# Handing the expert output to the MLP in on-chip memory, in expert order, in a fused attention, MoE and MLP kernel

## The chip, the cores and the metric

One Trainium2 chip, one core. The metric is the device time of one execution in microseconds (us), as the median of the timed runs. Engines: PE is TensorE (matmuls and transposes), ACT is ScalarE, DVE is VectorE, POOL is GpSimd, SP is SyncE. PEld is the weight load of TensorE, and a "q" behind an engine's name (ACTq) is its instruction sequencer, which works ahead of the engine.

## What is computed

```python
# x: (1152, 512), made by attention with queries averaged in pairs; batch b, position s is row 576*b + s
logits = x @ w_gate                       # 8 experts
e = argmax(logits); gate = softmax(logits)[e]
eom = sigmoid(x @ w_output_gate)[e]
y[e rows] = gate * eom * (relu(x[e rows] @ w1[e]) @ w2[e])      # w1: 512x1024, w2: 1024x512
h = y @ w_in                              # (1152, 2048)
out = (h * tanh(softplus(h))) @ w_out     # (1152, 512)
```

The dense MLP works on each row of `y` by itself, so the order of the rows is free as long as each result is written to its own row of `out`.

## The kernel before

**Attention** (up to about 290 us). Eight heads run in pairs, nine query tiles of 128 rows a head. The result, `x_tok`, is in token order. Meanwhile SP fills the DRAM buffer `slots_dram` with zeros and loads the weights of experts 0 and 1.

**Routing** (290 to 308.6 us). Logits, the chosen expert and each token's rank within its expert are worked out on PE and DVE. Every row is scaled by its gate and scattered by POOL (L677, one indirect DMA for each of the nine tiles) to its slot in `slots_dram`, where every expert begins on a tile boundary. DVE then works out how many tiles each expert has (`tile_end`, `bounds`) and at which row of `slots_dram` each tile lies (L1468 to L1476, `tile_rows`, semaphore `rows_ready`). After that it raises `h1_ready` (L1480), for which PE's first expert matmul waits. DVE's helper `then` lets each small operation wait for the one before it.

**Experts** (308.6 to 480.5 us). In this run 13 tiles of 128 slots are worked on, each with one expert's weights. `expert_tiles` (L451) is a loop of two groups of four experts, and inside it a loop over the tiles of each expert; four weight slots of 4 MB form the ring. Each step does:
- PE: first product into four PSUM banks, f = 0 to 7 (L995), then four transposes (`fill_xs`, L982) that turn the next tile, which lies in `stage`, into `turn[0]`, then the second product (L1009), f = 0 to 7, each f needing one eighth of w2 split into a high and a low part.
- ACT: ReLU to `hT_hi` (L1195) and the high part `w2_hi` (L1190) for f = 0 to 3 as they come, then `copy_xs` (L1179), then `w2_hi` for f = 4 to 7, then the DMA that loads `stage` for the tile after next (L1203).
- DVE: `hT_lo` (L1491), `w2_lo` (L1486), four of them late, and at the end the copy of the result to `y_sb` (L1500).
- POOL: writes `y_sb` back over the tile's own rows in `slots_dram` (L685) and waits for the landing.

SP loads each next expert when its ring slot is free (`wait_expert`, L578), then `w_in` (after expert 4) and `w_out` (after expert 5), 4 MB each.

**Hand-over** (480.5 to 518.5 us). When all tiles are stored, POOL gathers the rows back in token order, nine indirect DMAs (L691) into `x_tok`. ACT and DVE split `w_in` into high and low parts, four pieces of 2048 columns each (L1213, L1506). PE turns each gathered tile (`fill_x2`, L1020, four transposes), ACT and DVE split it into `x2T_hi` and `x2T_lo` (L1217, L1512). Three tiles come before the first MLP product, six between the first ones.

**MLP** (to the end). Three chunks of 384 rows, 16 steps each. A step f is `hidden` (L1032, 12 matmuls, run four steps ahead, `AHEAD`) and `project` (L1049, 9 matmuls). Between them lies the activation: ACT exp (L1222), ln (L1226), exp (L1228) and `g_hi` (L1234); DVE clip (L1520), L1522, L1539, L1542, L1534, L1548 and `g_lo` (L1527), which comes two DVE steps after its `hidden`. In chunk 0 each step also splits one sixteenth of `w_out` (L1256, L1576). PE's `hidden` waits for `h2_bank_free`, first raised by DVE at L1581. After a chunk, ACT (tiles 0 and 2) and DVE (tile 1) copy the result to `y_out`, and SP stores it (L603, L606; 128 KB twice for the last tile).

The lines on which the order hangs:

```python
            for n in range(RING):                      @@ SP
                wait_expert(n)
                load_expert(RING + n, n)
            wait_expert(RING)
            sp.dma_start(w_in_sb[:, :, :], w_in.rearrange("(t p) f -> p t f", p=P)).then_inc(w_in_landed, 16)
...
            pool.sem_inc(y_all_stored, 1)               # POOL
            pool.wait_ge(y_all_stored, 1)
            for i in range(TPH):
                pool.indirect_dma_start(x_tok[:, i, :], None, slots_dram,
                                        bass.IndirectOffsetOnAxis(slot_idx[:, i:i + 1], 0)).then_inc(y_back[i], 16)
```

Of the kernel before, what the change touches and what calls it, by code (L numbers as in the profile page):

```python
# [20 lines left out]
def build(nc, q, k, v, w_gate, w_ogate, w1, w2, w_in, w_out, out):  # L21
# [25 lines left out]
    XS_RING = 4  # L47
# [4 lines left out]
    DRAM_TILES = PAIRS * REGION // P  # L52
# [9 lines left out]
    FILL_STEPS = 3  # L62
# [9 lines left out]
    with ExitStack() as ctx:  # L72
# [18 lines left out]
        x_tok = sb("x_tok", [P, TPH, D], F32)  # L91
# [14 lines left out]
        row_step = sb("row_step", [P, NE], F32)  # L106
        row_base = sb("row_base", [P, NE], F32)
# [3 lines left out]
        tile_rows = sb("tile_rows", [P, ROW_TILES], I32)  # L111
        bounds = sb("bounds", [1, NE + 1], I32)
# [10 lines left out]
        parts_at = xsT_at + DT * N * 4  # L123
        ring = [ring_slot(n, at) for n, at in enumerate(ring_at)]

        w_in_sb = sb("w_in_sb", [P, DT, F2], F32, ring_at[0])
        w_in_lo = sb("w_in_lo", [P, DT, F2], F32R, ring_at[0])
        w_in_hi = sb("w_in_hi", [P, DT, F2], F32R, ring_at[2])
        w_out_sb = sb("w_out_sb", [P, FT2, D], F32, ring_at[1])
        w_out_lo = sb("w_out_lo", [P, FT2, D], F32R, ring_at[1])  # L130
        w_out_hi = sb("w_out_hi", [P, FT2, D], F32R, ring_at[3])
# [3 lines left out]
        xrT = sb("xrT", [P, DT, N], F32, ring_at[2])  # L135
        assert DT * N * 4 <= 2 * (B * KT * DH + TPH * 2 * DH) * 4
        x2T_hi = sb("x2T_hi", [P, DT, N], F32R, xsT_at)
        x2T_lo = sb("x2T_lo", [P, DT, N], F32R, xsT_at + DT * N * 4)
        stage = sb("stage", [P, FILL_AHEAD + 1, D], F32, xsT_at + DT * XS_RING * P * 4)

# [7 lines left out]
        y_out = sb("y_out", [P, TC, D], F32, x_tok_at)  # L148
        g_at = x_tok_at + TC * D * 4
        g_hi = sb("g_hi", [P, 2, CW], F32R, g_at)  # L150
        g_lo = sb("g_lo", [P, 2, CW], F32R, g_at + 2 * CW * 4)
        mish_at = [xsT_at + 2 * DT * N * 4]
# [15 lines left out]
        assert mish_at[0] <= top_at and g_at + 4 * CW * 4 <= x_tok_at + 2 * TC * D * 4  # L168

        small_from = xsT_at + DT * XS_RING * P * 4 + (FILL_AHEAD + 1) * D * 4  # L170
# [29 lines left out]
        row_of = small("row_of", [ROW_TILES, NE])  # L200
# [3 lines left out]
        raw_k = sb("raw_k", [P, 2, KT, B, DH], F32)  # L204
        raw_q = sb("raw_q", [P, 2, TPH, 2 * DH], F32)
# [8 lines left out]
        q_turned = sb("q_turned", [P, Q0 * P], F32)  # L214
        q_hi = sb("q_hi", [P, Q0 * P], F32R)
        q_lo = sb("q_lo", [P, Q0 * P], F32R)
        kT = sb("kT", [P, 2, B * S], F32R)
        qT_at = cursor[0]
        qT = sb("qT", [P, 2, 2, TPH * P], F32R)
        scratch = [sb(f"scratch{n}", [P, P], F32, x_tok_at + n * P * 4) for n in range(2)]  # L220
        prob = sb("prob", [P, 2, S], F32)
        probT = sb("probT", [P, 4, S], F32)
# [10 lines left out]
        assert qT_at <= small_from and small_at[0] <= qT_at + 2 * 2 * TPH * P * 4  # L233

        fill_bank = turn
        x2_fill_bank = [turn[0], turn[1], pvT]
# [40 lines left out]
        stage_landed = [sem(f"stage_landed{n}") for n in range(FILL_AHEAD + 1)]  # L277
# [7 lines left out]
        y_sb_free = sem("y_sb_free")  # L285
        s2_done = sem("s2_done")
        y1_copied = sem("y1_copied")
        y_stored = sem("y_stored")
        y_all_stored = sem("y_all_stored")
        y_back = [sem(f"y_back{n}") for n in range(TPH)]  # L290
        w_in_landed = sem("w_in_landed")
        w_out_landed = sem("w_out_landed")
# [8 lines left out]
        h2_bank_free = sem("h2_bank_free")  # L301
        g_ready = sem("g_ready")
        y2_done = sem("y2_done")
        y2_copied_act = sem("y2_copied_act")
# [390 lines left out]
        def _(pe):  # L695
# [364 lines left out]
            for i in range(TC):  # L1060
                fill_x2(i)
# [549 lines left out]
```

## Time and profile before

| | us |
|---|---|
| median of 3 runs | 721.02 (720.47 to 721.58) |
| profiled execution, its own time | 717.5 |
| its span (first to last instruction) | 715.9 |
| PE busy | 676.5 (94%) |
| DVE busy | 505.1 (71%) |
| ACT busy | 405.6 (57%) |
| POOL busy | 90.8 (13%) |
| mean granted clock of TensorE | 0.981 |

All positions in the trace are us from the start of the span. The profiled execution is 3.5 us shorter than the median of the runs. A duration printed for a matmul is longer than the distance to the next one, as matmuls overlap; the distance between starts is what they cost. Overlapping operations of DVE and ACT, too, follow each other some 0.07 to 0.09 us closer than their durations say.

### The profile page before, as it was taken

The numbers are of one execution on the slowest core, as the hardware profiler recorded it, in microseconds if no ns is written. First come the engines' busy times: TensorE is split into PE (matmuls) and PEld (weight loads), VectorE is DVE, ScalarE is ACT, GpSimd is POOL, SyncE is SP. The second block draws the span as 40 slices with busy tenths as digits, with TensorE's granted clock in tenths as the row PEclk, the third lists the DMA queues.
The fourth block names the chain that finished last, engine by engine and source line by source line (L and its number), as shares of the span: only waits on it lengthen the run. The fifth ranks groups of instructions, "written<-read, shape, count | busy, mean of one in ns | idle before, by whom it ended". The sixth has DMA issues, their size and how long they took to land.

```text
span 715.9 us, 14780 instructions
## 1 busy us (share of the span) xinstructions
PE 676.5 (94%) x5169; PEld 597.5 (83%) x5170; DVE 505.1 (71%) x1157; ACT 405.6 (57%) x810; POOL 90.8 (13%) x123
## 2 busy tenths in 40 slices
PE   5999999999999999989999999983799999999997
PEld 5788888888888888789998999973689998999895
DVE  5767676777677776756566566556899978777875
ACT  4657565756666667346555556653666645455442
POOL 2303040404041200320000000006000000000000
PEclk9899999999999999999999999995999999999999
DMA  7578989796977500389963991014000010001001
GB/s 190 142 204 221 279 206 262 172 260 153 256 165 203 133 3 1 99 310 402 399 246 121 349 347 47 29 48 128 15 1 1 1 44 1 1 0 45 1 1 44
DMA packets 92385, 99.00 MB, mean 138 GB/s; under 512 B 41584, under 2 KB 65136, under 8 KB 91824
## 3 DMA queue, kind: packets, MB, share of 16 engines
q1 hardware_dynamic: 87536, 86.22, 40.9%
q0 software_dynamic: 2480, 8.13, 3.2%
q10 hardware_dynamic: 2320, 4.00, 1.7%
q8 instruction: 30, 0.49, 0.3%
q14 instruction: 19, 0.16, 0.1%
HBM read 62.16 MB, written 19.66 MB: 114 GB/s over the span
## 4 chain that ended last, share of the span: by engine, by line
PE 89%; DVE 5%; ACT 2%; DMA 2%; issue 1%; POOL 1%; SPq 0%; ACTq 0%; POOLq 0%; DVEq 0%
PE score_banks L1032 14%; PE score_banks L995 13%; PE turn L782 12%; PE pvT L763 11%; PE score_banks L1009 10%; PE score_banks L739 5%; PE score_banks L740 5%; PE score_banks L1049 4%; PE turn L1049 4%; PE pvT L1049 4%; PE turn L703 1%; PE turn L982 1%; DMA raw_k<-k 1%; POOL x_tok L691 1%; PE turn L789 1%
## 5 line engine op out<-in xcount | busy, mean ns | idle before, releaser
L782 PE MATMUL turn<-ident,prob 128*128 128x128 f32 x648 | 111.5, 282 | 2.4 <-DVE x_tok L1330 0.5
L1277 DVE TENSOR_REDUCE nmax_part<-score_banks 128x1 f32<-128x768 f32 x72 | 68.9, 957 | 60.3 <-PE score_banks L740 46.9
L995 PEld LDWEIGHTS score_banks<-xsT,w_slot 128*128 128x128 f32 x832 | 94.6, 192 | 5.2 <-issue 4.2
L995 PE MATMUL score_banks<-xsT,w_slot 128*128 x832 | 95.2, 275 | 3.6 <-DVEq L1480 2.0
L782 PEld LDWEIGHTS turn<-ident,prob 128*128 128x128 f32 x648 | 77.5, 142 | 24.9 <-issue 14.0
L1078 ACT ACTIVATE prob<-score_banks,nmax 128x1152 f32<-128x1152 f32 x72 | 87.5, 1215 | 0.6 <-DVE nmax L1287 0.5
L1085 ACT ACTIVATE probT<-turn 128x384 f32<-128x384 f32 x72 | 35.4, 491 | 89.3 <-PE turn L782 89.3
L763 PE MATMUL pvT<-probT,v_sb 128*64 128x128 f32 (+1 forms) x1404 | 85.9, 269 | 0.0
L1486 DVE TENSOR_TENSOR w_lo<-w_slot,w_hi 128x512 fp32r<-128x512 f32 x104 | 71.7, 692 | 18.5 <-ACT w_hi L1190 18.4
L739 PE MATMUL score_banks<-kT,qT 128*128 128x384 f32 x192 | 80.1, 417 | 4.6 <-DVE qT L1306 3.9
L763 PEld LDWEIGHTS pvT<-probT,v_sb 128*64 128x64 f32 x1404 | 69.5, 137 | 11.8 <-issue 11.8
L1032 PE MATMUL score_banks<-x2T_hi,w_in_hi 128*128 128x384 f32 x192 | 66.1, 344 | 4.3 <-DVE x2T_lo L1512 4.3
L1195 ACT ACTIVATE hT_hi<-score_banks 128x128 fp32r<-128x128 f32 x104 | 28.8, 277 | 69.4 <-PE score_banks L995 64.6
L1190 ACT ACTIVATE w_hi<-w_slot 128x512 fp32r<-128x512 f32 x104 | 65.3, 628 | 2.1
L740 PE MATMUL score_banks<-kT,qT 128*128 128x384 f32 x192 | 65.7, 342 | 0.0
L1032 PE MATMUL score_banks<-x2T_hi,w_in_lo 128*128 128x384 f32 x192 | 65.5, 341 | 0.0
L1032 PE MATMUL score_banks<-x2T_lo,w_in_hi 128*128 128x384 f32 x192 | 65.2, 340 | 0.0
L1234 ACT ACTIVATE g_hi<-prod 128x384 fp32r<-128x384 f32 x48 | 25.3, 526 | 62.2 <-PE turn L1049 55.4
L1491 DVE SCALAR_TENSOR_TENSOR hT_lo<-score_banks,hT_hi 128x128 fp32r<-128x128 f32 x104 | 29.9, 287 | 30.0 <-ACT hT_hi L1195 30.0
L1527 DVE TENSOR_TENSOR g_lo<-prod,g_hi 128x384 fp32r<-128x384 f32 x48 | 26.7, 557 | 23.9 <-ACT g_hi L1234 22.3
L739 PEld LDWEIGHTS score_banks<-kT,qT 128*128 128x128 f32 x192 | 36.8, 192 | 7.1 <-DVE qT L1306 4.4
L1032 PEld LDWEIGHTS score_banks<-x2T_hi,w_in_hi 128*128 128x128 f32 x192 | 36.6, 191 | 7.0 <-DVE x2T_lo L1512 5.0
(218 smaller groups left out, 1358.0 us busy)
## 6 DMA issues: line engine op xcount, KB each, us to landing
w_slot<-moe_w SPq DMA_DIRECT2D x16, 2048.0 KB, 15.7
slots_dram<-zeros SPq DMA_DIRECT2D x8, 1408.0 KB, 11.1
raw_k<-k SPq DMA_DIRECT2D x16, 288.0 KB, 5.9
v_sb<-v SPq DMA_DIRECT2D x16, 288.0 KB, 4.3
w_in_sb<-moe_w_in SPq DMA_DIRECT2D x1, 4096.0 KB, 13.7
w_out_sb<-moe_w_out SPq DMA_DIRECT2D x1, 4096.0 KB, 14.6
kT<-k_hi SPq DMA_DIRECT2D x14, 288.0 KB, 4.3
kT<-k_lo SPq DMA_DIRECT2D x14, 288.0 KB, 5.2
```

The source lines that it names most:

```text
L739: pe.matmul(dst, parts(0, P), keys(b), start=True, stop=False)
L740: last = pe.matmul(dst, parts(1, P), keys(b), start=False, stop=True)
L763: last = pe.matmul(bank[half * DH:(half + 1) * DH, col:col + cols], v_sb[:, par, j, b, :], probT[:, pt_of[t], j * P + col:j * P + col + cols],
L782: last = pe.transpose(bank[:, j * P:(j + 1) * P], prob[:, s % 2, c * KC + j * P:c * KC + (j + 1) * P], ident[:, :])
L995: last = pe.matmul(h1_bank[f % 4][:, 0:P], w1_e[:, d, f * P:(f + 1) * P], xsT[:, d, bass.ds((t % XS_RING) * P, P)], start=(d == 0), stop=( ...
L1009: last = pe.matmul(y1_bank, h, w, start=(f == 0 and k == 0), stop=(f == FT1 - 1 and k == 2))
L1032: last = pe.matmul(h2_bank[f % 4][:, 0:CW], w, x, start=(d == 0 and k == 0), stop=(d == DT - 1 and k == 2))
L1049: last = pe.matmul(y2_bank[n], g, w, start=(f == 0 and k == 0), stop=(f == FT2 - 1 and k == 2))
L1078: act.activation(prob[:, s % 2, :].rearrange("p (c n) -> p c n", c=NC), scores[s % 2][:, :, 0:KC], ACT.Exp, bias=nmax[:, s:s + 1], accum_o ...
L1190: act.activation(w2_hi[:, f % W2_RING, :], ring[n][1][:, f, :], ACT.Copy).then_inc(w2_hi_ready, 1)
L1277: dve.tensor_reduce(nmax_part[:, s, 0:1], scores[s % 2][:, lo:lo + 2, 0:KC], AX.XY, ALU.max, negate=True).then_inc(max_part, 1)
L1486: dve.tensor_tensor(w2_lo[:, f % W2_RING, :], ring[n][1][:, f, :], w2_hi[:, f % W2_RING, :].bitcast(F32), ALU.subtract).then_inc(w2_lo_rea ...
```

## The change

After each expert tile the result `y_sb` is no longer written to DRAM. One tile later PE turns it (`turn_y`, four transposes into `turn[1]`), ACT and DVE split it into `x2T_hi` and `x2T_lo` at the column at which the tile's first row stands when all rows are sorted by expert (`tile_cols`); padding rows behind it are overwritten by the next tile. The MLP then runs on rows in expert order, and its results are scattered to the rows of `out` by POOL. The row numbers are worked out in chunk 1 of the MLP: DVE makes 0/1 matrices (`spread`), PE multiplies them with the row numbers (`gather_rows`, nine matmuls with nine columns), DVE copies them to `out_idx`. The experts are written out one by one. `w_in` and `w_out` are loaded in halves into the freed halves of four ring slots, and six of eight pieces of `w_in` (two 512-column stretches at a time) are split behind experts 5, 6 and 7, the last two in steps 0 and 1 of chunk 0. Raising `h2_bank_free` now stands on DVE behind the pieces that follow expert 7 and a register load of the number of tiles. In the routing, four operations of 128x144 elements and one reduction of these leave; seven of at most nine elements, four of 72, two of 288, one of 36, two small stores and the clearing of `y_sb` come, all ahead of `h1_ready`. At the start POOL makes six more small tables. In the last chunk ACT and DVE copy tiles 0 and 1 as soon as each is done (`y2_tile_done`). The loop over the MLP's middle chunk, which runs once, is written out.

```diff
-    XS_RING = 4
+    XS_RING = 2
...
+        first_pieces = {RING + 1: ((0, 0), (0, 1)), RING + 2: ((1, 0), (1, 1)), RING + 3: ((0, 2), (1, 2))}
+        late_pieces = ((0, 3), (1, 3))
+        PIECES_READY = (3, 4, 6, 8)
...
-            with eng.Fori(0, NE // RING) as grp:
...
+            for e in range(NE):
+                with eng.Fori(firsts[e], firsts[e + 1]) as t:
+                    body(t, e, look_ahead)
+                if behind is not None:
+                    behind(e)
@@ SP
-            sp.dma_start(w_in_sb[:, :, :], w_in.rearrange("(t p) f -> p t f", p=P)).then_inc(w_in_landed, 16)
...
+            for n in range(2):
+                wait_expert(RING + n)
+                sp.dma_start(w_in_sb[n][:, :, :], w_in_rows[:, n * HALF:(n + 1) * HALF, :]).then_inc(w_in_landed[n], 16)
+            for n in range(2):
+                wait_expert(RING + 2 + n)
+                sp.dma_start(w_out_sb[n][:, :, :], w_out_rows[:, n * HALF2:(n + 1) * HALF2, :]).then_inc(w_out_landed[n], 16)
@@ POOL
-            with pool.Fori(0, tiles) as t:
-                pool.dma_start(slots_dram[bass.ds(row, P), :], y_sb[:, :]).then_inc(y_stored, 16)
...
+            pool.wait_ge(order_ready, 1)
+            for i in range(TPH):
...
+                pool.indirect_dma_start(out, bass.IndirectOffsetOnAxis(out_idx[:, i:i + 1], 0),
+                                        y_out[:, i % TC, :], None).then_inc(out_landed, 16)
@@ PE
+            def turn_y(t):
+                pe.wait_ge(y1_copied, t + 1)
+                pe.wait_ge(x2_lo_ready, t + 1)
+                for d in range(DT):
+                    last = pe.transpose(x2_bank[:, d * P:(d + 1) * P], y_sb[:, d * P:(d + 1) * P], ident[:, :])
+                last.then_inc(x2_filled, 1)
...
                 pe.wait_ge(xs_copied, t + FILL_AHEAD)
...
-                pe.wait_ge(y1_copied, t + 1)
+                turn_y(t)
...
-            for i in range(TC):
-                fill_x2(i)
-            pe.wait_ge(x2_lo_ready, TC)
-            pe.wait_ge(win_lo_ready, DT)
-            for f in range(AHEAD):
-                hidden(0, f)
-                for i in later_fills[f]:
-                    fill_x2(i)
-            pe.wait_ge(x2_lo_ready, TPH)
+            pe.wait_ge(x2_lo_ready, tiles + 1)
+            hidden(0, 0)
+            turn_y(tiles)
+            for f in range(1, AHEAD):
+                hidden(0, f)
...
+                    if c == 1:
+                        for i in spread_in(f + 1):
+                            gather_rows(i)
@@ ACT
                 copy_xs(t + FILL_AHEAD, fill_bank[0], (t + FILL_AHEAD) % XS_RING)
+                x2_high(t)
                 for f in range(W2_RING, FT1):
                     w2_high(f)
...
+            def x2_high(t):
+                col = act.value_load(tile_cols[0:1, bass.ds(t, 1)], min_val=0, max_val=N)
+                act.wait_ge(x2_filled, t + 1)
+                act.activation(x2T_hi[:, :, bass.ds(col, P)], x2_bank[:, :].rearrange("p (d n) -> p d n", d=DT), ACT.Copy
+                               ).then_inc(x2_hi_ready, 1)
@@ DVE
+            dve.memset(y_sb[:, :], 0.0).then_inc(y1_copied, 1)
+            dve.sem_inc(x2_lo_ready, 1)
             dve.sem_inc(h1_ready, 4)
...
                 look_ahead(e)
+                x2_low(t)
                 for f in range(W2_RING, FT1):
                     w2_low(f)
                 dve.wait_ge(s2_done, FT1 * (t + 2))
-                dve.wait_ge(y_sb_free, t + 1)
+                dve.wait_ge(x2_filled, t + 1)
                 dve.tensor_copy(y_sb[:, :], y1_bank).then_inc(y1_copied, 1)
@@ PE, project
+                    if c == CHUNKS - 1 and f == FT2 - 1 and n < TC - 1:
+                        last.then_inc(y2_tile_done, 1)
```

## Rows read from the trace of the kernel before

**Rows 1.** Busy time by engine, granted clock and DMA in the stretch of the hand-over.

```profile
480.50:518.50 38.00, 19.00 (x98) 16.93 (x98) 26.29 (x37) 20.18 (x30) 13.05 (x10) 0.78 0.24 71
```

**Rows 2.** Timeline of PE, hand-over: start us, us, line, operation, [idle before <-releaser].

```profile
480.14 0.39 PE L1009 MATMUL score_banks<-w_hi,hT_lo 128*128 128x512 f32 x1
490.85 1.11 PE L1020 MATMUL turn<-ident,x_tok 128*128 128x128 f32 x4 [10.32 <-DMA x_tok<-slots_dram,slot_idx]
...
497.70 0.69 PE L1032 MATMUL score_banks<-x2T_hi,w_in_hi 128*128 128x384 f32 x1 [1.41 <-DVE x2T_lo L1512]
...
516.30 0.45 PE L1032 MATMUL score_banks<-x2T_hi,w_in_hi 128*128 128x384 f32 x1 [2.91 <-DVE x2T_lo L1512]
...
518.50 0.39 PE L1049 MATMUL score_banks<-w_out_hi,g_hi 128*128 128x512 f32 x1
```

**Rows 3.** Windows of 1 us in the hand-over; PEclk is the granted clock.

```profile
484.00:485.00 1.00, 0.00 (x0) 0.00 (x0) 1.00 (x1) 1.00 (x2) 0.00 (x0) 0.73 0.00 0
501.00:502.00 1.00, 1.00 (x7) 0.96 (x7) 0.00 (x0) 0.11 (x1) 0.00 (x0) 0.73 0.78 209
```

**Rows 4.** The chain that ended last: start us, us, what.

```profile
387.26 1.58 issue
...
485.40 3.11 POOL x_tok L691
```

**Rows 5.** Timeline inside one expert tile.

```profile
381.17 0.60 PE L982 MATMUL turn<-ident,stage 128*128 128x128 f32 x4
...
381.53 0.48 PE L1009 MATMUL score_banks<-w_hi,hT_hi 128*128 128x512 f32 x1
...
383.18 2.08 DVE L1486 TENSOR_TENSOR w_lo<-w_slot,w_hi 128x512 fp32r<-128x512 f32 x3 [1.20 <-ACT w_hi L1190]
...
384.38 0.39 PE L1009 MATMUL score_banks<-w_hi,hT_hi 128*128 128x512 f32 x1
```

**Rows 6.** Groups of instructions: out<-in, shapes xcount | busy us, mean ns | idle before.

```profile
L1506 DVE TENSOR_TENSOR w_in_lo<-w_in_sb,w_in_hi 128x2048 fp32r<-128x2048 f32 x4 | 8.9, 2286 | 1.8 <-ACT w_in_hi L1213 1.8
...
L1213 ACT ACTIVATE w_in_hi<-w_in_sb 128x2048 fp32r<-128x2048 f32 x4 | 7.3, 1897 | 2.7 <-DMA stage<-slots_dram 2.7
...
L1512 DVE TENSOR_TENSOR x2T_lo<-turn,x2T_hi 128x512 fp32r<-128x512 f32 x6 | 4.0, 686 | 3.3 <-ACT x2T_hi L1217 3.3
...
L1217 ACT ACTIVATE x2T_hi<-turn 128x512 fp32r<-128x512 f32 x6 | 3.4, 588 | 5.2 <-PE turn L1020 5.2
```

**Rows 7.** The line that loads a tile's row number into a register, on ACT's sequencer.

```profile
L1202 ACTq TENSOR_LOAD <-tile_rows x13: 278/279/288, 319.3 to 477.9; - x13
```

**Rows 8.** Timeline of DVE, first steps of the MLP.

```profile
502.42 0.36 DVE L1520 TENSOR_SCALAR expo<-expo 128x384 f32<-128x384 f32 x1 [4.77 <-ACT expo L1222]
...
511.76 0.35 DVE L1520 TENSOR_SCALAR expo<-expo 128x384 f32<-128x384 f32 x1
...
512.63 0.55 DVE L1527 TENSOR_TENSOR g_lo<-prod,g_hi 128x384 fp32r<-128x384 f32 x1
```

**Rows 9.** Groups on DVE in the routing.

```profile
L1474 DVE TENSOR_TENSOR row_of<-row_of,begun 128x144 f32<-128x144 f32 x1 | 0.3, 309 | 0.0
...
L1416 DVE SCALAR_TENSOR_TENSOR gain_inv<-picked,gate_sum 128x4 f32<-128x4 f32 (+1 forms) x2 | 0.3, 160 | 0.0
```

**Rows 10.** Timeline of PE at the start of the experts.

```profile
299.19 7.39 PE L937 MATMUL score_banks<-onehot,x_tok 128*128 128x128 f32 x64
308.60 0.59 PE L995 MATMUL score_banks<-xsT,w_slot 128*128 x3 [2.02 <-DVEq L1480]
```

**Rows 11.** Timeline at the end of the kernel.

```profile
711.08 0.60 ACT L1241 ACTIVATE y_out<-score_banks 128x512 f32<-128x512 f32 x1 [3.04 <-PE turn L1049]
...
712.55 1.18 SPq L606 DMA_DIRECT2D out<-y_out  x2
```

**Rows 12.** Issue to landing of the last tile's stores from SP, L606.

```profile
DMA to landing us min/median/max: 2.4/2.4/2.4
```

**Rows 13.** Issue to landing of the indirect DMAs from POOL, L691.

```profile
DMA to landing us min/median/max: 3.5/3.8/5.4
```

More of the change, by code:

```diff
@@ L276, in build @@
         xs_stored = sem("xs_stored")
-        stage_landed = [sem(f"stage_landed{n}") for n in range(FILL_AHEAD + 1)]
+        stage_landed = sem("stage_landed")
         xs_filled = sem("xs_filled")
@@ L1012, in _ @@
             expert_tiles(pe, pe_expert)
-            def fill_x2(i):
-                pe.wait_ge(y_back[i], 16)
-                if i >= 3:
-                    pe.wait_ge(x2_lo_ready, i - 2)
-                bank = x2_fill_bank[i % 3]
-                for d in range(DT):
-                    last = pe.transpose(bank[:, d * P:(d + 1) * P], x_tok[:, i, d * P:(d + 1) * P], ident[:, :])
-                last.then_inc(x2_filled, 1)
+            tiles = pe.value_load(bounds[0:1, NE:NE + 1], min_val=NE, max_val=SLOT_TILES)
             def hidden(c, f):
                 pe.wait_ge(h2_bank_free, FT2 * c + f + 1)
+                if isinstance(c, int) and c == 0 and f % RANGE == 0:
+                    pe.wait_ge(win_lo_ready, PIECES_READY[f // RANGE])
                 cols = bass.ds(c * CW, CW)
                 for d in range(DT):
-                    wh, wl = (w[:, d, f * P:(f + 1) * P] for w in (w_in_hi, w_in_lo))
+                    wh, wl = (w[d // HALF][:, d % HALF, f * P:(f + 1) * P] for w in (w_in_hi, w_in_lo))
                     xh, xl = x2T_hi[:, d, cols], x2T_lo[:, d, cols]
@@ L1247, in mlp_chunk @@
                     rough_recip(c, f)
-                    if first:
-                        for i in later_fills[f]:
-                            x2_high(i)
                     if f + 1 < FT2:
@@ L1260, in mlp_chunk @@
                         g_high(c - 1, FT2 - 1, False)
-            for i in range(TC):
-                x2_high(i)
-            act.wait_ge(w_out_landed, 16)
             h2_exponential(0, 0)
+            x2_high(tiles)
             for c in range(CHUNKS):
@@ L1393, in sign_slots @@
                 tiles, count = slice(batches[n].start, batches[n].stop), len(batches[n])
-                then(dve.tensor_tensor(signed[:, tiles, :], chosen[:, tiles, :], spread(slot_sign[:, :], count, NE), ALU.mult))
+                then(dve.tensor_tensor(signed[:, tiles, :], chosen[:, tiles, :], spread_over(slot_sign[:, :], count, NE), ALU.mult))
             def pick(n):
@@ L1551, in copy_y @@
             def copy_y(c):
-                dve.wait_ge(y2_done, FT2 * (c + 1))
+                if c == CHUNKS - 1:
+                    dve.wait_ge(y2_tile_done, 2)
+                else:
+                    dve.wait_ge(y2_done, FT2 * (c + 1))
                 dve.wait_ge(y_out_free, c + 1)
@@ L1559, in mlp_chunk @@
                     mish_numer(c, f)
+                    if first and not f:
+                        x2_low(tiles)
                     if f >= 2:
```

355 lines of the change are left out of this document (215 added, 140 removed).

## The prediction, made before the changed kernel was run

> **What bounds the kernel now.** I read the busy shares first: PE is at 94%, so time is to be found where PE waits. The busy time by stretch shows one place: in the 38.0 us of the hand-over PE is busy for 19.0, at a mean clock of 0.78 [rows 1]. The timeline of PE tells what it waits for [rows 2]. The last expert matmul starts at 480.14, the first transpose of a gathered tile at 490.85, after 10.32 us that ended with a DMA; the first MLP matmul starts at 497.70, the first `project` at 518.50. Stand-alone windows show the clock: 0.73 from 484 to 485, so it fell from 2.4 to 1.2 GHz some 0.5 us into that window, 3.9 us after the last matmul ended at 480.53; again 0.73 from 501 to 502, so it rose near 501.5, after 3.8 us of dense matmuls [rows 3]. Elsewhere PE works back to back, in the experts and in the MLP, and everything added to PE there counts in full. The chain of waits adds two things [rows 4]: POOL's first gather (3.11 us), and 1.58 us of "issue" at 387.26, after the sixth expert tile, where the loop over groups of experts jumps back.
>
> **What the change removes, up to the first `project`.** I build its new start from the front.
>
> *Start of the experts.* PE ended at 299.19 + 7.39 = 306.58 and waited until 308.60 for DVE's `h1_ready` [rows 10]. That increment now stands behind more routing work. By the groups on DVE [rows 9] an operation of a few elements takes 0.16 and one of 144 takes 0.31, each about 0.04 more with its wait; so 0.20, about 0.26 for 72 elements, 0.50 for 288, 0.24 for 36. Added: 7 x 0.20 + 4 x 0.26 + 2 x 0.50 + 0.24 + 0.2 for two small stores = 3.9. Removed: 5 x 0.35 = 1.7. Sum **+2.2** (1.7 to 2.9; the upper end if the clearing of `y_sb` must end, too, at L1512's length [rows 6]). The six POOL tables cost nothing: the first use of the tables is hundreds of us later, and POOL's next work at the start waits for a DMA; without that cover, six small operations are 1.2.
>
> *Transposes.* `fill_xs` takes 381.53 - 381.17 = 0.36 for its four [rows 5]; `turn_y` has the same four, in 13 tiles: **+4.7**. Its input was copied a whole first product before, so PE doesn't wait for it. Behind it, ACT's x2 split (0.59) and DVE's (0.69) [rows 6] now stand ahead of the late parts of w2. The cover: the first late `w2_lo` starts at 383.18 and takes 0.69, done at 383.87; PE needs it at 384.38 [rows 5]. That is 0.51 minus some semaphore time, say 0.45. `turn_y` gives PE's need 0.36 more. ACT's part delays the split by 0.59; DVE's then ends just behind ACT's next w2 part. About 0.2 us of cover is left, so I cost it at nothing. The column load into a register (0.28 [rows 7]) can run while `copy_xs` runs; if not, it uses that cover up.
>
> *Loop written out.* The jump back between the groups goes: **-1.6** (0 if something else, such as loading code, takes its place).
>
> *Pieces of w_in.* A split of 2048 columns takes 1.90 on ACT and 2.29 on DVE [rows 6]; between the 512 and the 2048 rows, 1024 takes 1.05 and 1.22. After experts 5 and 6 DVE does two of them (2.4) at the head of the next tile. PE's fifth bank use waits for the first `hT_lo` only four products later, 3.6 us; that nearly covers it: **+0.2** (0 to 0.8). The loads of 2 MB have a whole tile to land.
>
> So the last expert matmul's slot, 480.37 before, ends at 480.37 + 2.2 + 4.7 - 1.6 + 0.2 = 485.9.
>
> *First MLP product.* PE now needs only `h2_bank_free`. ACT's two pieces end about 0.7 after the last product; DVE's sequencer then queues the last split, loads the number of tiles (0.28 plus handling) and raises it. I take 1.6 (0.6 if only the load counts; 3.5 if `y_sb`'s copy and both splits had to end first). First `hidden` at 487.5.
>
> *From there to `project`.* A `hidden` at full clock takes 518.50 - 516.30 = 2.2 [rows 2]. Then come 0.1 and ACT's exp, about 0.6 by the nearest row, to DVE's clip: 2.9. From the first clip to the end of the first `g_lo` it was 512.63 + 0.55 - 502.42 = 10.8 [rows 8]. In these two steps four x2 splits (4 x 0.69) go, one (0.69) and two pieces of w_in (2 x 1.22) come, +0.4, and each piece waits for ACT's 1.05 where a 0.59 stood, +0.8. So 2.9 + 10.8 + 1.2 + 0.1 = 15.0 and `project` starts at 502.5, not 518.50: **-16.0**. Here PE has only five `hidden` and one `turn_y` to do, 11 us, and waits 4.0; the DVE chain is the late one now.
>
> **What it adds behind.** *Row numbers:* nine small matmuls with a full weight load each; L937 has 64 such pairs in 7.39, 0.115 each [rows 10], so **+1.0** (0.4 to 1.7). DVE's part is hidden, since DVE is 71% busy and two steps ahead. *Last store:* SP issued the second part of the last tile at about 713.14, and it landed 2.4 later [rows 11, 12], 4.5 us after the copies began at 711.08. Now the third indirect DMA starts at about 712.95 (POOL, 1.25 apart, from the first copy, which comes some 0.7 earlier, three matmuls of 0.24 [rows 5]), and lands 3.5 later [rows 13]: **+0.9** (-0.4 if POOL is free at the last copy, +2.8 at the longest landing). A page speaks against moving this: the Trainium skill, "DMA: Bandwidth & Descriptors", section "Specifications", gives about 1 us to the first byte for a DMA issued by GpSimd and 0.6 from the sync path. By its difference alone the last landing would be 0.4 later, where the rows here make it 1.1.
>
> **Clock.** PE now waits 4.2 us before the first expert product (306.58 to 310.8) and 4.0 before the first `project`. The only fall in a wait here came after 3.9. A fall costs half of 3.8 us = 1.9. Both waits lie at the edge; I count one fall: **+1.9** (0 to 3.8).
>
> **Sum.** -16.0 + 1.0 + 0.9 + 1.9 = -12.2 against the profiled execution's 717.5 us: 705.3. The median shown is 3.5 us above that execution; against it, 721.0 - 12.2 = **708.8 us**.
>
> **The rivals.**
> - *Half clock at both edges, or a longer chain.* The trace speaks for it with the half clock from 484.5 to 501.5; against it, waits of 2.02 and 2.91 us [rows 2, 10] before matmuls at full speed. Two falls: 710.7. With the first product released only at 3.5, another 1.9: 712.6. The Trainium skill, "TensorE: Matmul & The Clock Gate", section "HAM oscillation — how this bites in real kernels", has every repeated wait for data throttle the array again and charges half of the throttled time; by that rule this is the likely outcome, and the one fall seen here agrees with it.
> - *No fall, and the DVE chain shorter than laid out.* 706.9 without a fall; down to 703 if the pieces of w_in overlap the activation better than I have it.
> - *Code loading.* If the 1.58 us stays although the loop is gone, 710.4. If each new expert's code costs it, 7 x 1.58 more, 721. Against it: experts 1 to 3 were entered for the first time without a wait in the chain.
> - *Slower.* In every tile the two x2 splits stand between `copy_xs` and the late w2 parts. If the register loads aren't hidden (0.28 and as much handling on each queue), and both splits lie in the chain in full, that is 0.59 + 0.69 + 1.2 = 2.5 against a cover of 0.45 + 0.36 = 0.8: 1.7 a tile, 13 tiles, +22, so 731. It decides from 12.2/13 = 0.94 us a tile. Against it: the two queues run beside each other, and DVE is idle for 1.20 ahead of the first late `w2_lo` [rows 5].
> - *It doesn't do what it says.* If the MLP's start were held by the splits of w_in or the activation chain as long as before, the gather's wait would have been cover only, and the 7 us added would show: 722 or so. Against it: 10.32 us of the wait end with the DMA [rows 2].
>
> **How the numbers follow.** Forecast, one fall give or take half of one: 0.48. Both falls or a longer chain, 710.5 to 714: 0.22. Better, 703 to 707: 0.19. Code loading of a part: 0.04. Slower: 0.04. No real effect: 0.03. The first three give the range, 703.0 to 714.0, which also takes in the bounds of start (+0.7), release (+1.9) and landing (+1.9) one at a time. A measurement of this kernel can tell about 0.2% (1.4 us) from no change. Faster by more than that 0.93, within 0.02, slower 0.05.
>
> **What would show it.** In the changed profile: the first L995 matmul near 310.8; each tile 0.36 longer than before, with no wait of PE between `turn_y` and the second product; no "issue" after the sixth tile; the first MLP product 1.6 us after the last expert one; then about 4 us of waiting for `g_lo` and `project` at 503 to 505; nine small matmuls in chunk 1 without waits; about 5.4 us from the last matmul's release to the end. Wrong would be: tiles over 0.94 longer, a wait of over 4 us before the first MLP product, or more than two stretches at half clock.

## The result, and the profile after

The changed kernel takes **710.27 us** (median of 4 runs, 709.43 to 712.92) beside 721.3 us for the kernel before: 11.0 us less, a ratio of 0.9848 [0.9814, 0.9882]. The forecast was 708.8 with a range of 703.0 to 714.0, so sign and time were right. Its case, one fall of the clock, was not: there are two. The time came out by luck: terms that were too small by 6.5 us in all were made up for by the executions that the sum was measured against. The rest of this text takes that apart.

| | before | changed |
|---|---|---|
| profiled execution, own time | 717.5 | 712.92 |
| its span | 715.9 | 711.2 |
| mean granted clock | 0.981 | 0.988 |
| last expert matmul starts | 480.1 | 492.9 |
| first `hidden` | 497.7 | 494.4 |
| first `project` | 518.5 | 509.4 |

The head of the page, changed kernel (share of the span):

```profile
PE 681.7 (96%) x5207; PEld 601.9 (85%) x5207; DVE 509.8 (72%) x1193; ACT 408.2 (57%) x819; POOL 80.9 (11%) x115
```

PE has 5 us more work than before and the kernel is shorter all the same. The timeline of PE, changed kernel, at the start of the experts and in the hand-over (start us, us, instruction, [idle before <-releaser]), answers to [rows 2, 10]:

```profile
312.82 0.79 PE L1035 MATMUL score_banks<-xsT,w_slot 128*128 x2 [3.95 <-ACT xsT L1218]
...
494.41 0.41 PE L1066 MATMUL score_banks<-x2T_hi,w_in_hi 128*128 128x384 f32 x1 [1.16 <-DVEq L1596]
...
509.45 0.76 PE L1083 MATMUL score_banks<-w_out_hi,g_hi 128*128 128x512 f32 x1 [3.93 <-DVE g_lo L1607]
510.01 0.63 PE L1083 MATMUL score_banks<-w_out_lo,g_hi 128*128 128x512 f32 x1
```

The wait of 10.32 us for the gathered rows is gone; what is left before the first MLP product is 1.16 us, until DVE's register load, and the DVE chain to `g_lo` is the late one from there on, as laid out: 15.04 us from the first `hidden` to the first `project`. The windows of the changed kernel (the column behind POOL's is the granted clock) show what the two long waits bring:

```profile
310.00:311.00 1.00, 0.00 (x0) 0.00 (x0) 0.93 (x3) 0.00 (x0) 0.99 (x1) 1.00 1.02 414
311.00:312.00 1.00, 0.00 (x0) 0.00 (x0) 0.86 (x8) 0.09 (x1) 0.13 (x1) 0.60 1.04 422
312.00:313.00 1.00, 0.18 (x1) 0.19 (x2) 0.76 (x3) 0.51 (x1) 0.00 (x0) 0.50 0.86 348
...
317.00:318.00 1.00, 1.00 (x7) 1.00 (x6) 0.77 (x2) 0.43 (x1) 0.00 (x0) 0.50 0.85 252
318.00:319.00 1.00, 1.00 (x11) 1.00 (x11) 0.44 (x2) 0.73 (x2) 0.00 (x0) 0.99 0.87 242
...
509.00:510.00 1.00, 0.55 (x1) 0.50 (x2) 1.00 (x3) 0.97 (x3) 0.00 (x0) 0.59 0.00 0
510.00:511.00 1.00, 1.00 (x4) 0.80 (x3) 1.00 (x3) 0.93 (x3) 0.00 (x0) 0.50 0.00 0
...
512.00:513.00 1.00, 1.00 (x4) 0.76 (x4) 0.96 (x3) 0.33 (x1) 0.00 (x0) 0.71 0.00 0
513.00:514.00 1.00, 1.00 (x7) 0.96 (x7) 1.00 (x4) 0.97 (x3) 0.00 (x0) 1.00 0.00 0
```

Both waits of about 4 us let the clock fall from 2.4 to 1.2 GHz: at the start of the experts it stays down until 318 (11 matmuls a us instead of 7 from there), at the first `project` until about 512.6. The 17 us at half clock of [rows 3] are gone.

One tile, changed kernel (timeline), answers to [rows 5]:

```profile
390.86 0.60 PE L1013 MATMUL turn<-ident,stage 128*128 128x128 f32 x4
391.30 0.60 PE L1022 MATMUL turn<-ident,y_sb 128*128 128x128 f32 x4
391.65 0.47 PE L1049 MATMUL score_banks<-w_hi,hT_hi 128*128 128x512 f32 x1
...
392.37 0.60 ACT L1232 ACTIVATE x2T_hi<-turn 128x512 f32 x1
392.86 2.45 ACT L1241 ACTIVATE w_hi<-w_slot 128x512 fp32r<-128x512 f32 x4
...
393.12 0.69 DVE L1556 TENSOR_TENSOR x2T_lo<-turn,x2T_hi 128x512 f32 x1 [1.45 <-ACT x2T_hi L1232]
393.72 2.48 DVE L1564 TENSOR_TENSOR w_lo<-w_slot,w_hi 128x512 fp32r<-128x512 f32 x4
...
394.26 0.39 PE L1049 MATMUL score_banks<-w_hi,hT_lo 128*128 128x512 f32 x1
394.55 0.47 PE L1049 MATMUL score_banks<-w_hi,hT_hi 128*128 128x512 f32 x1
394.86 0.39 PE L1049 MATMUL score_banks<-w_lo,hT_hi 128*128 128x512 f32 x1
```

`fill_xs` to `turn_y` is 0.44 here, not 0.36, `turn_y` to the second product 0.35. The 13th matmul of the second product comes 0.29 behind the 12th and the 14th 0.31 behind that, where nearly all others are 0.23 apart: the first late `w2_lo`, 393.72 to 394.4, is just too late. So the cover of the x2 splits had not 0.2 us left but was 0.06 short, and being 0.06 short costs 0.14. The chain of the changed kernel around that tile:

```profile
383.88 7.14 PE score_banks L1035 x64
391.03 0.44 PE turn L1013 x4
391.46 0.44 PE turn L1022 x4
391.90 5.65 PE score_banks L1049 x24
397.55 7.14 PE score_banks L1035 x64
```

Tile follows tile after 13.67 us (13.07 before), with no piece of "issue" between them, behind the sixth either. That 1.58 us [rows 4] is gone.

The routing on DVE, changed kernel, with ACT's first copy:

```profile
307.42 0.16 DVE L1521 CAST bounds<-tile_end 1x9 int32<-1x9 f32 x1
...
309.84 0.46 DVE L1535 TENSOR_TENSOR begins_at<-begun,starts_of 128x288 f32<-128x288 f32 x1
310.33 0.45 DVE L1537 TENSOR_REDUCE tile_at_f<-begins_at 128x36 f32<-128x288 f32 x1
...
312.15 0.16 DVE L1547 TENSOR_TENSOR out_row_f<-out_row_f,tail_part 128x1 f32<-128x1 f32 x1
312.48 0.48 DVE L1549 MEMSET y_sb<- 128x512 f32 x1 [0.17 <-DVE out_row_f L1547]
...
311.91 0.60 ACT L1218 ACTIVATE xsT<-score_banks 128x512 f32<-128x512 f32 x1 [11.32 <-remote]
```

One of the row products in chunk 1, and the end of the kernel (timeline of the changed kernel):

```profile
583.99 0.39 PE L1083 MATMUL turn<-w_out_hi,g_lo 128*128 128x512 f32 x1
584.22 0.28 PE L1091 MATMUL turn<-rows_by_tile,spread 128*128 128x9 f32 x2
584.36 0.42 PE L1066 MATMUL score_banks<-x2T_hi,w_in_hi 128*128 128x384 f32 x1
584.61 0.34 PE L1066 MATMUL score_banks<-x2T_lo,w_in_hi 128*128 128x384 f32 x1
...
703.13 0.60 ACT L1298 ACTIVATE y_out<-score_banks 128x512 f32<-128x512 f32 x1 [1.71 <-PE score_banks L1083]
...
704.00 0.96 POOL L721 DMA_INDIRECT out<-y_out,out_idx  x1 [54.81 <-ACT y_out L1298]
...
705.27 0.96 POOL L721 DMA_INDIRECT out<-y_out,out_idx  x1 [0.30 <-issue]
706.53 0.96 POOL L721 DMA_INDIRECT out<-y_out,out_idx  x1 [0.30 <-issue]
```

Each fp32 product of nine columns is two passes (x2), and delays the work behind it by 584.61 - 584.22 - 0.18 = 0.21 us. At the end POOL is the bound, 1.26 us a DMA, and the third one needs another 4.7 us to the end of the span at 711.2.

### The profile page after: what moved, and what is told of

It is laid out like the page before. It is cut to its first block, busy times and chain, and to the rows that moved or that the text cites. A ratio compares the mean times of both kernels' runs of the same rounds, so it can differ in the third digit from the quotient of the medians.

```text
span 711.2 us, 14872 instructions
## 1 busy us (share of the span) xinstructions
PE 681.7 (96%) x5207; PEld 601.9 (85%) x5207; DVE 509.8 (72%) x1193; ACT 408.2 (57%) x819; POOL 80.9 (11%) x115
## 4 chain that ended last, share of the span: by engine, by line
PE 89%; DVE 4%; ACT 2%; another core or an unknown queue 2%; issue 1%; DMA 1%; POOL 0%; DVEq 0%; SPq 0%; ACTq 0%
PE score_banks L1035 13%; PE score_banks L1066 13%; PE turn L813 11%; PE pvT L794 11%; PE score_banks L1049 10%; PE score_banks L770 5%; PE score_banks L1083 5%; PE score_banks L771 5%; PE pvT L1083 4%; PE turn L1083 4%; PE turn L734 1%; DMA raw_k<-k 1%; PE turn L1022 1%; PE turn L1013 1%
## 5 line engine op out<-in xcount | busy, mean ns | idle before, releaser
L1035 PEld LDWEIGHTS score_banks<-xsT,w_slot 128*128 128x128 f32 x832 | 97.1, 196 | 5.2 <-issue 4.1
L1035 PE MATMUL score_banks<-xsT,w_slot 128*128 x832 | 97.5, 279 | 3.9 <-ACT xsT L1218 3.9
L794 PEld LDWEIGHTS pvT<-probT,v_sb 128*64 128x64 f32 x1404 | 69.5, 137 | 11.9 <-issue 11.9
L1564 DVE TENSOR_TENSOR w_lo<-w_slot,w_hi 128x512 fp32r<-128x512 f32 x104 | 68.2, 687 | 3.0 <-ACT w_hi L1241 2.9
L1241 ACT ACTIVATE w_hi<-w_slot 128x512 fp32r<-128x512 f32 x104 | 63.5, 625 | 0.7
L721 POOL DMA_INDIRECT out<-y_out,out_idx x9 | 8.9, 991 | 387.4 <-DVE out_idx L1688 308.9
L1049 PE MATMUL score_banks<-w_hi,hT_hi 128*128 128x512 f32 x104 | 42.8, 411 | 0.0
```

The lines of the kernel that those rows point to most:

```text
L794: last = pe.matmul(bank[half * DH:(half + 1) * DH, col:col + cols], v_sb[:, par, j, b, :], probT[:, pt_of[t], j * P + col:j * P + col + cols],
L1035: last = pe.matmul(h1_bank[f % 4][:, 0:P], w1_e[:, d, f * P:(f + 1) * P], xsT[:, d, bass.ds((t % XS_RING) * P, P)], start=(d == 0), stop=( ...
L1049: last = pe.matmul(y1_bank, h, w, start=(f == 0 and k == 0), stop=(f == FT1 - 1 and k == 2))
L1241: act.activation(w2_hi[:, f % W2_RING, :], ring[n][1][:, f, :], ACT.Copy).then_inc(w2_hi_ready, 1)
L1564: dve.tensor_tensor(w2_lo[:, f % W2_RING, :], ring[n][1][:, f, :], w2_hi[:, f % W2_RING, :].bitcast(F32), ALU.subtract).then_inc(w2_lo_rea ...
```

## The experiments

Each ratio is against the kernel before, run beside the experiment. The first four (the kernel without the gather, late pieces, splits behind, no row products) ran on one chip, the others in two sets on another. No changed kernel ran beside the first four; I compare them with its 710.27 of the result, whose chip is not on record (the kernel before took 721.3 us beside it and 721.05 beside the four), so differences of 1 to 2 us there are weak. The others have a repeat of the changed kernel beside them, 709.47 and 710.51.

**The gather alone.** The kernel before without its nine gathers; `x_tok` keeps what it held, so the MLP works on other rows of data, in the same shapes.

```diff
-            for i in range(TPH):
-                pool.indirect_dma_start(x_tok[:, i, :], None, slots_dram, ...)
...
-                pe.wait_ge(y_back[i], 16)
...
+            dve.wait_ge(y_all_stored, 1)
             dve.sem_inc(h2_bank_free, 4)
```

> The kernel before without the nine gathers and without PE's wait for them: the MLP gets the scaled inputs in token order instead of the experts' output; the stores of the expert output stay. Theory (the round trip is only a part; the splits of w_in and their place on ACT and DVE are the next bound): DVE ends the last w_in split where it did, about 11.5 us after the last expert matmul, then does three x2 splits, so the first MLP matmul comes about 13.6 us after the last expert matmul instead of 17.2, and the kernel is 3 to 4 us faster than before (717 to 718 against 721). Rival (the round trip is the whole of the 10.3 us wait and its clock): first MLP matmul within 5 us, 10 to 13 us faster.

Measured: 719.77 us (10 runs), ratio 0.9982 [0.9962, 1.0002]: 1.3 us less, by the interval between 2.7 less and no gain, although 10.32 us of waiting ended with those gathers. That is also less than the 3 to 4 us expected. Its timeline:

```profile
497.95 0.69 PE L1028 MATMUL score_banks<-x2T_hi,w_in_hi 128*128 128x384 f32 x1 [12.14 <-DVE x2T_lo L1508]
```

The wait moved to DVE, which had the splits of `w_in` ahead of the x2 splits. The first `hidden` comes 13.8 us after the last expert matmul instead of 17.6, as expected, but from it to `project` it is 22.4 instead of 20.8, with one more stretch at half clock behind a wait of 2.99 us: the hand-over is 2.1 us shorter in all. **The gather was a cover for the splits of w_in,** and taking it away alone brings next to nothing.

**The other half alone.** The changed kernel with all six early pieces of `w_in` behind expert 7.

```diff
-first_pieces = {RING + 1: ((0, 0), (0, 1)), RING + 2: ((1, 0), (1, 1)), RING + 3: ((0, 2), (1, 2))}
+first_pieces = {RING + 3: ((0, 0), (0, 1), (1, 0), (1, 1), (0, 2), (1, 2))}
```

> The changed kernel with all six early pieces of w_in split behind expert 7 instead of behind experts 5, 6 and 7. Theory: four more pieces on ACT (about 0.96 us each) stand ahead of the release of the first MLP matmul, so PE waits about 1.1 + 4 = 5 us there instead of 1.1, with a fall of the clock on top (1.7 to 2): 4 to 6 us slower than the changed kernel, which was 710.3. Rival (w_in's splits don't matter, the removal of the round trip alone made the gain): within 1 us of it.

Measured: 715.15 us (5 runs), ratio 0.9921 [0.9891, 0.9951], 4.9 over the changed kernel.

```profile
497.07 0.66 PE L1066 MATMUL score_banks<-x2T_hi,w_in_hi 128*128 128x384 f32 x1 [4.94 <-DVEq L1596]
```

The wait before the first `hidden` is 3.8 longer, and its products run at half clock: 16.85 instead of 15.04 us to `project`. So the gain of the change is made of both parts: rows that stay on chip, and pieces of `w_in` that are split under the experts.

**x2 splits behind the late w2 parts**, on ACT and DVE.

```diff
                 copy_xs(t + FILL_AHEAD, fill_bank[0], (t + FILL_AHEAD) % XS_RING)
-                x2_high(t)
                 for f in range(W2_RING, FT1):
                     w2_high(f)
+                x2_high(t)
```

> The changed kernel with the two x2 splits of each expert tile moved behind the late parts of w2 on ACT and DVE. Theory (the tile costs 0.61 us more than before, 0.36 of it the four transposes, and the rest because the late w2 parts come later than PE needs them): the gap of 0.31 between the 12th and 13th matmul of the second product falls back to 0.23, a tile takes 13.07 + 0.36 to 13.07 + 0.45, and the kernel is 2 to 3 us faster than the changed one. Rival (the extra 0.25 is PE's own cost of two transposed tiles in a row with their waits): 13.65 a tile, no change.

Measured: 710.25 us (4 runs), ratio 0.9853 [0.9835, 0.9871]. The tile is 13.49 instead of 13.66 and the gap in it is gone, so the x2 splits did cost 0.17 a tile where they stood. But the two tiles that begin with pieces of `w_in` on ACT and DVE take 13.75, and behind the last tile the splits now delay the last pieces:

```profile
490.67 0.41 PE L1066 MATMUL score_banks<-x2T_hi,w_in_hi 128*128 128x384 f32 x1 [2.08 <-DVEq L1596]
```

From the second tile to the last expert matmul 1.6 us come in (not 13 x 0.17 = 2.2), and 0.9 go out; the median shows no difference from the changed kernel's. In the pair with and without the move that the other chip ran (below) it is -2.0.

**No row products** (the results are then written in expert order, not to their own rows; the nine 0/1 matrices on DVE are left out, too).

```diff
-                        for i in spread_in(f + 1):
-                            gather_rows(i)
...
-                    dve.tensor_copy(out_idx[:, :], x2_bank[:, 0:TPH])
+                    dve.tensor_copy(out_idx[:, :], out_row_f[:, :])
```

> The changed kernel without the nine 0/1 matrices and the nine products; the results are scattered by the unsorted row numbers, so rows of the output land in other places, with the same stores. Theory: each product costs PE 0.19 us; the nine steps of chunk 1 take 4.19 instead of 4.39 us, 1.7 us less in all. Rival (the products fill gaps that stay): no change in the steps.

Measured: 708.72 us (4 runs), ratio 0.9839 [0.9815, 0.9863]. From the first `project` to the last matmul it is 192.7 us beside 194.6 with the products: 1.9 for nine, 0.21 each.

**The changed kernel again**, as yardstick.

> The changed kernel once more, beside the next three: 709.4 to 712.9 were measured. Its first expert tile took 16.4 us instead of 13.3 in the trace of before, and so did the kernels of the first call, the one built on the kernel before too (15.7): theory, the half clock at the start of the experts is common to both kernels in most runs. Then this trace shows it again (a first tile of 15.5 us or more). Rival: it was chance, and some traces show 13.7.

Measured: 709.47 us (5 runs), ratio 0.988 [0.9852, 0.9909]; kernel before 718.21 (11 runs).

```profile
311.58 2.71 PE L1035 MATMUL score_banks<-xsT,w_slot 128*128 x11 [3.78 <-DVEq L1551]
```

ACT's copy was done at 308.4 here, and the wait ends with the increment at the end of the routing, 5.3 us after `bounds` (3.5 before). The first tile takes 16.48 us, the later ones about 13.66: **the fall costs 2.8 us** in this profile.

**The release right behind the bounds.**

```diff
             dve.tensor_copy(bounds[0:1, :], tile_end[0:1, :]).then_inc(bounds_ready, 1)
+            dve.sem_inc(h1_ready, 4)
...
+            dve.sem_inc(rows_ready, 1)
             dve.memset(y_sb[:, :], 0.0).then_inc(y1_copied, 1)
...
-            dve.sem_inc(h1_ready, 4)
@@ ACT
-            act.wait_ge(rows_ready, 1)
+            act.wait_ge(rows_ready, 2)
```

> The changed kernel with the release of the first expert product right behind the tile counts, some 4.7 us earlier in DVE's work; ACT waits for the rest of the routing instead, before it writes over the small tables. Theory (DVE's longer routing is the bound of the start): PE starts the experts about 0.3 us after ACT's first xsT copy, 2 to 3 us earlier after the tile counts than the 5.3 us of the changed kernel, and if the wait falls under 3 us the clock doesn't fall (2.4 more): 2 to 5 us faster than the changed kernel. Rival (ACT's late copy of the first tile, which the trace puts down to an unknown queue, is as late as DVE): PE starts less than 0.5 us earlier, no change.

Measured: 706.24 us (6 runs), ratio 0.984 [0.9814, 0.9867], 3.2 less than the changed kernel beside it.

```profile
307.85 3.83 PE L1035 MATMUL score_banks<-xsT,w_slot 128*128 x32 [1.37 <-ACT xsT L1218]
...
311.68 0.28 ACT L1246 ACTIVATE hT_hi<-score_banks 128x128 fp32r<-128x128 f32 x1 [4.57 <-PE score_banks L1035]
...
312.33 4.07 PE L1035 MATMUL score_banks<-xsT,w_slot 128*128 x32 [0.66 <-DVE hT_lo L1570]
```

PE starts 2.9 us after `bounds`, behind ACT's copy, and the clock stays at 1.00. Yet the first tile takes 15.15 us, not 13.66. The edit also makes ACT wait for the end of the routing (`rows_ready`); ACT loads the tile counts only from 310.1 on and begins `hT_hi` at 311.68. PE has filled its four banks by then and waits for the `hT_lo` behind it. So 2.4 us come from the earlier start and 1.3 from the first tile, and 0.35 are lost in the third tile (14.00; why stays open): 3.4 in all, near the 3.2 of the medians. The longer routing still costs time in this version, through ACT.

**The same, with the load of the next w1 held back** until the first copy is done, to see if that load makes ACT's copy late.

```diff
+            sp.wait_ge(xs_copied, 1)
```

> The kernel with the early release, and with the 2 MB load of expert 2's first weights held back on SP until ACT has copied the first tile. Theory (ACT's first xsT copy is late by 2 to 3 us because what it waits for, its instructions by the look of it, comes by DMA behind that load and the scatters): ACT copies within 0.3 us of the last product of the placing, PE starts the experts about 1 us after it, at full clock: a first tile of 13.7 us, and 4 to 5 us faster than the changed kernel. Rival (the lateness has nothing to do with the load): ACT is as late as before, the same time as the kernel with the early release alone.

Measured: 711.03 us (6 runs), ratio 0.9905 [0.988, 0.9931]. ACT's copy came right behind the last product of the routing, but so it did beside it without this wait: no answer. The run is 4.8 us slower. In its profile, 2.6 of that lie between `bounds` and the second tile, as the load of `stage` now lands late and PE waits 2.35 us for it, and 1.3 at the first `project`, where the clock stays at half for 6.8 us instead of 3.4.

**A warm clock at the first project:** 18 matmuls more, whose result nobody reads, while PE waits for `g_lo`.

```diff
+                    if first and f == 0:
+                        pe.wait_ge(x2_lo_ready, tiles + 2)
+                        for _ in range(18):
+                            pe.matmul(x2_bank[:, 0:CW], w_in_hi[0][:, 0, 0:P], x2T_hi[:, 0, 0:CW], start=True, stop=True)
                     project(c, f, first)
```

> The changed kernel with 18 more matmuls of 384 columns (their result is not used) between PE's fifth hidden product and the first project, 3.1 us in the 3.9 us that PE waits there. Theory (the half clock at the first project comes from that wait): it stays at full clock, the first project takes 2.1 instead of 3.6 us, 1.5 us faster than the changed kernel. Rival (the clock falls for another reason, or the added matmuls push the project back): no gain, or up to 0.5 us slower.

Measured: 707.31 us (5 runs), ratio 0.9853 [0.9824, 0.9883], 2.2 less than the changed kernel beside it.

```profile
505.30 0.47 PE L1083 MATMUL score_banks<-w_out_hi,g_hi 128*128 128x512 f32 x1 [0.83 <-DVE g_lo L1611]
```

The first `project` takes 2.1 us instead of 3.6: 1.5, as expected, which shows that the fall there comes from the wait. The rest of the gain need not be the edit's. Counted from `bounds` to the end, this profile is 2.6 us shorter than that of the changed kernel, and 1.05 of it lies in the first expert tile (15.43 instead of 16.48, same order of work), where the clock happened to come back sooner.

**Put together.** The yardstick, then early release and warm clock, then these and the splits behind.

> The changed kernel once more, as the yardstick of this call. Expected 709.5 +- 1 by the median, first tile of the experts 16.4 to 16.7, tiles of 13.66 after it, first hidden matmul to first project matmul 15.0.

> The release right behind the bounds and the matmuls that keep the clock, together. If the two costs are separate, the gains add: 3.2 and 2.2 below the changed kernel of the same call, so about 704.1. If one only uncovers the other (a fall that is avoided at one place comes at the next), it stays at 706 to 707.

> As the run with the early release and the kept clock, and the splits of x2 behind those of w2 as well. By my reading the tiles shrink from 13.66 to 13.49 (13 x 0.17 = 2.2) and the first hidden matmul waits 1.1 longer: net 1.1 below the kernel without the move. The rival: the wait grows by as much as the tiles give, and the two are equal within 0.3.

Measured, with the kernel before at 717.25 beside them (9 runs):

| | us (runs) | ratio to before |
|---|---|---|
| changed again | 710.51 (5) | 0.9906 [0.9889, 0.9923] |
| early, warm | 706.40 (4) | 0.9859 [0.9839, 0.9878] |
| early, warm, splits behind | 704.38 (5) | 0.9821 [0.9804, 0.9839] |

Early release and warm clock bring 4.1 us by the medians, between the 3.2 of the first alone and the 5.4 of both added. The profiles tell more: from `bounds` to the end the pair is 4.9 us shorter than the changed kernel, which is 3.4 for the release and 1.5 for the warm `project`, so the two add up. The profile of this pair has no half clock from the start of the experts to the last matmul. The version with all three beats both kernels of this case: 6.1 us under the changed one, 2.0 under the pair. Its profiled execution had no luck at one place; its timeline and its windows there:

```profile
487.76 0.41 PE L1066 MATMUL score_banks<-x2T_hi,w_in_hi 128*128 128x384 f32 x1 [2.08 <-DVEq L1601]
```

```profile
487.00:488.00 1.00, 0.24 (x1) 0.27 (x2) 1.00 (x2) 0.01 (x1) 0.00 (x0) 1.00 0.75 186
488.00:489.00 1.00, 1.00 (x5) 1.00 (x5) 0.67 (x1) 0.00 (x0) 0.00 (x0) 0.57 0.79 150
489.00:490.00 1.00, 1.00 (x5) 1.00 (x4) 0.00 (x0) 0.00 (x0) 0.00 (x0) 0.50 0.96 326
```

The same wait of 2.08 us that let the clock be in the run with the splits behind alone was followed by a fall here, and `project` came 16.6 us after the first `hidden` instead of 15.0.

## Why the prediction was right, and where its terms were off

The sum was made against a profiled execution of 717.5 us, so it is checked against one of the changed kernel with the same start of the attention, that of the first repeat (span 710.2; 715.9 before). Each row is a distance between two events in the two traces:

| stretch | before | changed | found | predicted |
|---|---|---|---|---|
| start to `bounds` | 305.1 | 306.3 | +1.2 | 0 |
| `bounds` to first expert matmul | 3.5 | 5.3 | +1.8 | +2.2 |
| first tile | 13.2 | 16.5 | +3.3 | +0.4, and +1.9 once for a fall |
| the other tiles, to the last matmul | 158.4 | 163.8 | +5.4 | +2.9 |
| to the first `hidden` | 17.6 | 1.6 | -16.0 | -15.7 |
| to the first `project` | 20.8 | 15.0 | -5.8 | -5.8 |
| to the last matmul | 192.1 | 194.6 | +2.5 | +1.0 |
| to the end | 5.3 | 7.2 | +1.9 | +0.9 |
| sum | | | -5.7 | -12.2 |

- **What made the kernel faster was right to 0.3 us:** the hand-over (-21.8 for -21.5). The release after the register load came out as summed (1.56 for 1.6), and so did the chain of DVE in its parts: 2.96 to the first clip (2.9), 11.9 from there to the end of the first `g_lo` (12.0).
- **Start of the experts.** +1.8 for +2.2, within its bounds. That clearing `y_sb` must end was wrong: in the changed kernel PE's first matmul starts at 312.82, with the MEMSET under way until 312.96.
- **Transposes, the term that was mis-sized most.** 0.60 a tile instead of 0.36, so 13 x 0.60 = 7.8 for 4.7. 0.08 lies between `fill_xs` and `turn_y`, 0.14 to 0.17 at the second product's late matmul. The step that failed is "about 0.2 us of cover is left, so I cost it at nothing": moving the splits away gave back 0.17 a tile, so the cover was used up. It also shows that the rival "slower" had the right place; it needed 0.94 a tile and got 0.60.
- **Loop written out.** -1.6 was right: no "issue" is left between the tiles, and no other piece took its place; the rival of code loading is out. The +0.2 for the pieces of `w_in` was not needed: the tiles behind them take 13.66 and 13.68, like the others.
- **Clock.** "Both waits lie at the edge; I count one fall" is the step that failed. Both fell in every profile of the unaltered changed kernel: 2.6 to 2.8 us in the first tile and 1.5 at `project` (its first step takes 5.7 us instead of 4.2), 4.3 for the 1.9 of the forecast. The rival "half clock at both edges" (0.22) names what happened, with 710.7 against the 710.27 measured. The rule of the Trainium skill, "TensorE: Matmul & The Clock Gate", section "HAM oscillation — how this bites in real kernels", that every repeated wait throttles again, gave the outcome here where I rated it as the less likely; the runs bound it from the other side, since waits of 1.16, 1.37 and 2.35 us let the clock be.
- **Row products.** 1.9 for 1.0. The sum took a single pass of 0.115 each; each product is two, and the matmul behind them is late too. Without them the stretch is 1.9 us shorter.
- **Last store.** +1.9 for +0.9. The third DMA starts 2.5 after the last matmul (2.35 forecast; two slips cancel there: against the last matmul the first copy came 1.34 earlier than before, not 0.7, since six matmuls and not three lie behind its tile, and the 0.6 that the copy itself takes were left out). It needs about 4.3 to land (an estimate: 4.7 less the 0.4 that lay between landing and end before), not the 3.5 taken from [rows 13]. The difference to SP's 2.4 is 1.9. "DMA: Bandwidth & Descriptors" of the Trainium skill, section "Specifications", gives 1 us and 0.6 us to the first byte for the two paths, 0.4 apart. Here the stores differ in size and kind as well (256 KB indirect, 128 KB plain), so no run shows what share of the 1.9 is the path's.
- **Not foreseen.** MLP steps take 4.186 us instead of 4.207, 48 of them -1.0; why stays open. `bounds` came 1.2 to 2.3 us later than before in the three profiles of the unaltered changed kernel, but not in most of the edited ones (303.4 to 306.2), so I take it for scatter between executions.

By this table the sum was 6.5 us too hopeful, and yet 708.8 stands 1.5 from the measured median. The rest is the yardstick. The profiled execution of the kernel before was 3.5 us under its median, and those of the changed kernel 1.7 to 2.7 over theirs. The kernel before and the changed kernel side by side show why the first may be so:

| | before | changed | difference |
|---|---|---|---|
| with the result | 721.3 | 710.27 | -11.0 |
| first four experiments | 721.05 | - | - |
| next set, other chip | 718.21 | 709.47 | -8.7 |
| last set, that chip | 717.25 | 710.51 | -6.7 |

In all four profiles of the first experiments ACT's first `xsT` copy starts 3.8 to 4.9 us after `bounds`, released by something outside the trace, and so it does in the changed kernel's first profile (4.5); in all seven of the two later sets, and in that of the kernel before, it starts after 1.5 (2.5 where the w1 load is held back). In the order of before, where the routing releases PE after 3.5 us, a late copy is the bound: the kernel without the gather started its experts 5.8 us after `bounds`, and its first tile took 15.57 us instead of 13.16, 4.7 us lost in all. In the changed kernel the longer routing holds PE 5.3 us in any case (5.4 and 5.5 in the profiles with the latest copies). The profiled 717.5 us are what the kernel before takes on the other chip. That fits a kernel before that is 3 to 4 us slower on the one chip, and a changed one that is not; but the chip was not varied for one kernel's profile, so it is argued, not shown.

## What to carry to other kernels

A wait that ends with a transfer is worth only what is late next: ask which engine had queued work under it, as the gather's 10.3 us were worth 1.3 until the splits of `w_in` had gone from there as well. Take the time of a stage from starts on both sides of it, in every profile: what looks like a clean gain can hide a wait for the next engine in line, as ACT's did behind the early release. Work that is added to a chain in front of the first matmul of a stage costs its own time and then the clock; raise the semaphore as soon as what the consumer reads is ready, and where a wait of 4 us can't be avoided, idle matmuls pay for themselves. Cover of 0.2 us that is worked out from rounded gaps is none, and against a single profiled execution a sum is only as good as that execution stands to the median.

## What the runs showed of the hardware that was not expected

- **The length of a wait alone doesn't tell if the clock falls.** Waits of 2.99 us and more always ended in half clock, waits of up to 1.6 never. Between them both happens: after 2.91 before a `hidden` the kernel before went on at full clock [rows 2], without its gathers it fell at the same place after 2.99; 2.02 [rows 10] and 2.35 (for `stage`) let the clock be; and the wait of 2.08 before the first `hidden` was followed by a fall in one execution and by none in another, in the same order of work there. Nor does the fall come at a fixed time: at the start of the experts the clock fell at 311.2, 2.3 us after PE's last matmul, at `project` 3.7 us after it.
- **The fall can come after the work has begun again:** in the version with all three, PE took up at 487.76 with the clock at 1.00, and the windows show 0.57 and 0.50 from 488 on. It is not rare: with the early release alone PE took up the first `project` at 503.71, and the window from 504 to 505 shows 0.85, that from 505 to 506 shows 0.50.
- **What a fall costs changes with chance.** At the start of the experts the clock came back 5.1 to 6.2 us after PE's first matmul in six profiles, and the first tile took 2.5 to 3.1 us more than the others; in the two others, with the warm `project` and without the row products, it came back after 3.8 and 4.2 us and the tile took 1.7 to 1.8 more. At the first `project` of the unaltered changed kernel the first step took 1.5 us more (5.7 instead of 4.2), with the w1 load held back 2.9 (7.08). The windows of the profile with the warm `project`, whose experts start at 309.53:

```profile
309.00:310.00 1.00, 0.47 (x4) 0.48 (x4) 0.64 (x2) 0.00 (x0) 0.00 (x0) 0.96 0.89 361
...
313.00:314.00 1.00, 1.00 (x9) 1.00 (x9) 0.45 (x2) 0.80 (x2) 0.00 (x0) 0.84 0.73 223
```

- **Two releasers can lie so close that the profile names now one, now the other:** where ACT's copy came 4.5 us after `bounds`, PE started 5.4 and 5.5 us after it and the wait is put down to the copy; where the copy was earlier, PE started at 5.3 and it is put down to DVE's queue.
